# Seven unit loads begin during memory clearing, and the preparation of units in the first four pairs is dealt out anew

## The reference

```
for t in range(S):                                   # S = 768
    y[:, :, t] = einsum('bhd,bhde->bhe', r_t, state)
    Sa = einsum('bhde,bhe->bhd', state, a_t)
    state = state * w_t - outer(Sa, b_t) + outer(v_t, k_t)
x = y as (3072, 320)
g = h - tanh(h), h = x @ w_in (320 x 2048);   x = g @ w_out
out = sum over e of p[:, e] * (relu(x @ w1[e]) @ w2[e]),  p = probs / sum(probs)
```

## Time and profile before

| what | us |
|---|---|
| median of 3 runs | 1708.87 |
| the runs | 1700.08 to 1709.82 |
| the profiled execution | 1711.34 |
| its span on the core | 1709.6 |

### The profile page before, as it was taken

One profiled execution on the slowest core, in us unless ns is written; L12 is line 12 of the kernel. 1 busy time (PEld: TensorE's weight loads), 2 busy tenths in 40 slices (PEclk: granted clock), 3 DMA queues, 4 the chain that ended last, 5 costly groups with the idle time before them and its releaser, 6 DMA issues. The chain is left out here.

```text
span 1709.6 us, 37877 instructions
## 1 busy us (share of the span) xinstructions
PE 1494.2 (87%) x15888; PEld 1296.8 (76%) x15888; DVE 805.4 (47%) x1395; ACT 423.2 (25%) x859; POOL 403.9 (24%) x362
## 2 busy tenths in 40 slices
PE   0278476988989998899996969999999999999998
PEld 0266355876877786697795859999999999999998
DVE  5767844956855675493411133333333333333332
ACT  0023233333323323332432221111111111111111
POOL 5122354324323332231133341201010101010000
PEclk9988677999997998998998979999999999999999
DMA  7645475057046307403101051010101010100011
GB/s 196 195 107 148 131 221 163 4 144 210 27 105 172 104 5 200 109 5 99 27 1 35 10 167 34 0 34 0 34 0 34 0 34 0 34 0 0 0 46 46
DMA packets 83483, 123.06 MB, mean 72 GB/s; under 512 B 10016, under 2 KB 61472, under 8 KB 83360
## 3 DMA queue, kind: packets, MB, share of 16 engines
q1 hardware_dynamic: 83360, 121.27, 25.5%
HBM read 83.84 MB, written 37.40 MB: 71 GB/s over the span
## 5 line engine op out<-in xcount | busy, mean ns | idle before, releaser
L1330 PE MATMUL banks<-x2t,u 128*128 x1536 | 377.4, 393 | 8.6 <-POOL u L1297 8.6
L1340 PE MATMUL banks<-u,hid 128*128 128x320 f32 x2304 | 360.6, 309 | 0.0
L1340 PEld LDWEIGHTS banks<-u,hid 128*128 128x128 f32 x2304 | 349.0, 188 | 11.2
L1330 PEld LDWEIGHTS banks<-x2t,u 128*128 128x128 f32 x1536 | 284.1, 189 | 61.5 <-issue 8.8
L1395 DVE SCALAR_TENSOR_TENSOR hid<-banks,hid 128x512 fp32r<-128x512 f32 x192 | 132.8, 692 | 413.9 <-ACT hid L1365 413.9
L1365 ACT ACTIVATE hid<-banks 128x512 fp32r<-128x512 f32 x192 | 115.0, 599 | 581.5 <-PE banks L1330 581.5
L763 PE MATMUL banks<-xt,wi 128*128 128x512 f32 x768 | 197.0, 400 | 19.8 <-issue 12.4
L772 PE MATMUL banks<-wo,hid 128*128 128x320 f32 x1152 | 183.8, 309 | 5.7 <-POOL hid L1167 5.7
L772 PEld LDWEIGHTS banks<-wo,hid 128*128 128x128 f32 x1152 | 175.3, 188 | 14.1 <-POOL hid L1167 6.4
L763 PEld LDWEIGHTS banks<-xt,wi 128*128 128x128 f32 x768 | 142.3, 191 | 47.6 <-issue 21.0
L1167 POOL TENSOR_TENSOR hid<-gap,hid 128x512 fp32r<-128x512 f32 x96 | 123.7, 1288 | 223.5 <-ACT hid L903 223.2
(11 more groups left out here) (105 smaller groups left out, 1635.9 us busy)
## 6 DMA issues: line engine op xcount, KB each, us to landing
scaled_operands<-made SPq DMA_DIRECT2D x42, 520.8 KB
made<-kbaw SPq DMA_DIRECT2D x42, 520.0 KB
kb<-scaled_operands SPq DMA_DIRECT2D x24, 416.0 KB
raw<-w SPq DMA_DIRECT2D x8, 640.0 KB, 5.7
lam<-scaled_operands SPq DMA_DIRECT2D x24, 209.6 KB
raw<-w SPq DMA_DIRECT2D x8, 512.0 KB, 4.0
rt<-rvt SPq DMA_DIRECT2D x96, 40.0 KB
vt<-rvt SPq DMA_DIRECT2D x96, 40.0 KB
```

Of the source, the lines that this page charges most:

```text
L1330: mm = pe.matmul(p_up[f][:], u1[:, par, w, f * 128:(f + 1) * 128], xt[:, x, cols], start=(i == 0), stop=(i == 7))
L1340: mm = pe.matmul(p_dn[t][:, 0:D], hid[:, f, h, t * 128:(t + 1) * 128], u2[:, par, w, f, :], start=(f == 0 and i == 0), stop=(f == NFU - 1 ...
```

## The change

**Loads during clearing.** SP gets a program in the first block: the raw loads of units 0 to 6, in place of the loads of units 0 to 4 that stood at the head of `start`. Units 5 and 6 go into the memory of `nvmak` and of `kbn`, which their own stages write first in `mask_scores(0, 0)` and `save_natural(0, 0)`. These two therefore wait, the first time, until unit 5 or unit 6 has been stored. DVE clears a constant column in both.

**Slots.** Units 0 to 6 have slots of their own. Then a ring of five is used up to unit 16, and one of three from 17 on. In `start` SP now loads units 7 to 14 (before: 5 to 12).

**Preparation.** Pair 0 prepares units 10 to 13 and pair 1 prepares 14 and 15 (before: three each). Pairs from 3 on are as before.

**Inverse of chunk 1.** Its steps in pairs 2 and 3 are (0, 6, 7, 4, 6) and (3, 2, 6, 4, 6), 44 in all (before: (2, 3, 3, 2, 4) in each, 28 in all). The other 22 (before: 38) run after pair 3.

**Weight pieces.** `PIECES_FROM` is 4, so the pieces come in pairs 4 to 7 (before: 3 to 6), and `load_tokens(0)` moves behind the last pieces of pair 7 on SP.

```diff
+EARLY = RING + 2
-PIECES_FROM = 3
+PIECES_FROM = 4
+LAST_RAW = (15, 16)

 def slot(i):
-    return i % RING if i < 2 * NG else i % MADES
+    if i < EARLY:
+        return i
+    return (i - EARLY) % RING if i <= LAST_RAW[1] else (i - LAST_RAW[1] - 1) % MADES
...
 def prepared_in(p):
     if p < 2:
-        return list(range(FIRST + 3 * p, FIRST + 3 * p + 3))
+        return [[10, 11, 12, 13], [14, 15]][p]
 def loaded_in(p):
-    if p < 3:
-        return [[13, 14], [15], [16]][p]
+    if p < 4:
+        return [[], [15], [16, 17], [18]][p]
...
+            @block.sync
+            def _(sp):
+                for i in range(EARLY):
+                    sp.dma_start(raw_of(i)[0:PR, 0:WW + OP_LAM], kbaw[i, :, :]).then_inc(raw_op_in[i], 16)
...
             def start():          # SP
-                for i in range(RING):
-                    load_raw(i)
...
-                    if 0 < i <= 8:
-                        load_raw(i - 1 + RING)
+                    if 0 < i <= RING:
+                        load_raw(i - 1 + EARLY)
+                    if i >= 8:
+                        load_raw(i + 4)
+                load_raw(14)
...
             def pair(p):          # SP
-                if p == 2 * PPC - 1:
-                    load_tokens(0)
-                elif p % PPC == 0 and p >= 2 * PPC:
+                if p % PPC == 0 and p >= 2 * PPC:
                     load_tokens(c - 1)
...
                     raw_piece(2 * (p - PIECES_FROM) + 1)
+                if p == 2 * PPC - 1:
+                    load_tokens(0)
...
             def save_natural(p, j):
+                if p == 0 and j == 0:
+                    act.wait_ge(op_stored[RING + 1], 16)
             def mask_scores(p, j):
+                elif j == 0:
+                    dve.wait_ge(op_stored[RING], 16)
...
             def pair(p):          # DVE
-                spread = PPC - 2 <= p < PPC
+                steps = {2: (0, 6, 7, 4, 6), 3: (3, 2, 6, 4, 6)}.get(p, (0, 0, 0, 0, 0))
...
+                if p == 0:
+                    invert_decay(i[0])
                 sides(1)
+                if p == 0:
+                    prepare(i[1])
...
                 sides(2)
+                if p == 0:
+                    prepare(i[2])
...
+                if p == 0:
+                    prepare(i[3])
                 some(4)
                 update_state(p)
-                for k in i[2:]:
-                    prepare(k)
```

More of the change, by code:

```diff
@@ L186, in raw_of @@
             t = slot(i)
-            return made[:, t, :] if t < MADES else spare[:, t - MADES, :]
+            if t < MADES:
+                return made[:, t, :]
+            if t < RING:
+                return spare[:, t - MADES, :]
+            if t == RING:
+                return nvmak[:, :, :, :, :, :].rearrange("p j s a q t -> p (j s a q t)")[:, 0:MADE]
+            return kbn[:, :, :, :, :, :].rearrange("p k j a q e -> p (k j a q e)")[:, 0:MADE]
         def parts(i):
@@ L240, in _ @@
                     dve.memset(t[:, :, WW + OP_LAM::C + 1], 1.0).then_inc(set_v, 1)
+                for i in range(RING, EARLY):
+                    dve.memset(raw_of(i)[:, WW + OP_LAM::C + 1], 1.0).then_inc(set_v, 1)
                 dve.memset(rt[:], 0.0).then_inc(set_v, 1)
@@ L243, in _ @@
                 dve.memset(un[:], 0.0).then_inc(set_v, 1)
-                dve.wait_ge(set_v, 5)
+                dve.wait_ge(set_v, 7)
             @block.gpsimd
@@ L263, in _ @@
                 pool.wait_ge(set_p, 9)
-        raw_op_in = [sem(f"raw_operands_loaded{i}") for i in range(RING)]
-        op_stored = [sem(f"operands_stored{i}") for i in range(RING)]
+        op_stored = [sem(f"operands_stored{i}") for i in range(EARLY)]
         kb_in = [sem(f"scaled_kb_loaded{i}") for i in range(2)]
@@ L408, in raw_piece @@
                 if i < 2:
-                    last = 13 + i
+                    last = LAST_RAW[i]
                     sp.wait_ge(op_stored[slot(last)], 16 * uses(last))
@@ L1045, in pair, with some @@
                 finish = p > 0 and not drained(p - 1)
-                spread = PPC - 2 <= p < PPC
-                def some(n):
-                    if spread:
-                        inverse_steps(1, n)
+                steps = {2: (0, 6, 7, 4, 6), 3: (3, 2, 6, 4, 6)}.get(p, (0, 0, 0, 0, 0))
+                def some(k):
+                    inverse_steps(1, steps[k])
                 def sides(b):
@@ L1061, in pair @@
                     mask_ur(p - 1)
-                some(2)
+                some(0)
+                if p == 0:
+                    invert_decay(i[0])
                 sides(1)
-                for k in i[:1]:
-                    invert_decay(k)
-                some(3)
+                if p == 0:
+                    prepare(i[1])
+                elif i:
+                    invert_decay(i[0])
+                some(1)
                 sides(2)
@@ L1069, in pair @@
                     save_result(p - 1)
-                for k in i[1:2]:
-                    scan(k, 0)
-                    scan(k, 1)
-                some(3)
+                if p == 0:
+                    prepare(i[2])
+                elif i:
+                    scan(i[1], 0)
+                    scan(i[1], 1)
+                some(2)
                 sides(3)
@@ L1076, in pair @@
                     mask_scores(p + 1, 0)
-                some(2)
+                some(3)
                 if p + 1 < NP:
                     mask_scores(p + 1, 1)
-                for k in i[1:2]:
-                    invert_decay(k)
+                if p == 0:
+                    prepare(i[3])
+                elif i:
+                    invert_decay(i[1])
                 some(4)
                 update_state(p)
-                for k in i[2:]:
-                    prepare(k)
             def make_gap(c, f):
```

5 lines of the change are left out of this document (2 added, 3 removed).

## The result

The changed kernel takes **1712.89 us** (median of 20 runs, 1707.91 to 1724.46); the kernel before, on the same chip and in the same rounds, 1708.65 (20 runs, 1692.44 to 1718.61). The ratio is **1.0044, with a 95% interval from 1.0027 to 1.0062**: slower by some 7.5 us (the two medians by themselves lie 4.2 apart), and within the 1% that the prediction called no change. The profiled execution took 1712.49 us, its span is 1710.8.

What follows compares the result with a forecast made beforehand. It took the first MLP matmul's start as decisive, with the load queue pacing the start and DVE's inverse the stretch after pair 3; -15.2 + 16.4 = +1.2 us gave 1712.5 profiled, 1710 beside the median, range 1698 to 1720.

Steps and rivals of the forecast that it cites:

- 1, the start: Start: earlier raw loads, with two more in the queue, let the first mask begin at 49.8 instead of 51.03; -1.3 us.
- term 2: Pair 0: a fourth preparation comes in, two now lying between block rows where DVE waited for PE anyway; +0.1 us.
- term 3: Pair 1: the 3.7 us preparation behind its state update goes, one more diagonal passes through PE; -2.5 us.
- term 4: Pair 2: DVE's 2.78 us wait for a diagonal's copy goes, nine added inverse steps meet idle time; -3.0 us.
- 5, pair 3 and the tail: Pair 3 and the inverse behind it: added steps lengthen the pair, the tail loses 12.6 us; together -8.5 us.
- 6, pieces and tokens: Before the first MLP: pair 7's weight pieces and the tokens' load behind them delay its first matmul; +16.4 us.
- B: Rival, start: the queue is quicker than measured, engines set the pace, mask at 38.6; 1699 us, chance 0.12.
- C: Rival, pair 2: added inverse steps stand on the chain, losing its gain and costing up to 3 more; 1715, chance 0.17.
- D: Rival, start: no data moves before the first block ends, so the mask starts 3.9 us later; 1715, chance 0.09.

Runs made afterwards that it cites:

- e6: Changed kernel with units 2 and 3 instead of 5 and 6 loaded into the mask's and natural keys' memory; ratio to the kernel before 1.0035.
- e9: Kernel before with only its own five raw loads moved into the first block, during clearing; ratio to the kernel before 0.9923.
- e12: Kernel before with its five raw loads begun during clearing and the changed numbers of inverse steps; 1696.29 us, ratio to the kernel before 0.9921.
- e4: Changed kernel with its seven raw loads put back behind the clearing of memory, at the head of `start`; ratio to the kernel before 1.0080.
- e3: Changed kernel with the old numbers of inverse steps, 14 each in pairs 2 and 3; ratio to the kernel before 1.0104.
- e10: Changed kernel with pair 2's small loads of r issued ahead of its store and raw loads; ratio to the kernel before 1.0016.
- e1: Changed kernel with the weight pieces begun in pair 3 again instead of pair 4; ratio to the kernel before 1.0008.
- e2: Kernel before with only the weight pieces begun in pair 4 and the tokens' load behind them; ratio to the kernel before 1.0064.
- e11: e7 with the order of pair 2's transfers from e10; ratio to the kernel before 0.9914.
- e7: Changed kernel with the edits of e1 and e6 together; ratio to the kernel before 0.9955.

## Why the prediction was right, by its steps

The prediction had a gain of 15.2 us up to pair 4, paid back by 16.4 at the MLP. The trace has 11.4 and 15.5.

*1, the start (-1.3): right.* Measured -0.73 at the mask and at the inverse. The mechanism was the named one: the store of unit 5 had to leave the mask's memory, and the wait is longer than the 1.3 suggests, since without it the mask could have started at 39.57, 10.7 us sooner; e6 gives back 5.6 of them. The prediction put the early issue at 3.75 us. Held against all traces with the same start, it is 3.7 to 5.0 with five loads (e9, e12) and 2.5 to 3.7 with seven (e4).

*2 to 4, pairs 0 to 2 (together -5.4): mis-sized.* Measured, from each pair's start to the next, -2.5, +1.1 and 0.0, together -1.4. The failing steps are 3 and 4: they miss 6.6 us, and it is luck that term 2, forecast at +0.1, hides 2.6 of it.

In term 3 I took the 3.7 us of preparation behind a state update for time on the chain. They weren't. Without them pair 1 starts 3.7 sooner behind pair 0's update (0.63 against 4.32 us), which is the gain that term 2 shows, but from update to update it takes 23.90 us, 23.36 before. And pair 2 takes 22.01 in e12, where that preparation still stands behind pair 1's update, and 21.3 to 22.2 in the kernels without it. Pair 0 itself grew by 1.2 (from its start to its update 17.67 against 16.51), so the preparations between its block rows were not free. In pair 1 PE's waits for nothing that the profile shows also went from 2.50 us in one place to 3.65 in two; the prediction had no term for them.

In term 4 the nine added steps were to fall into DVE's idle time. They stand on the chain: from the mask of the second block row to the state update pair 2 takes 14.00 us, 11.86 before, and DVE waits for no other engine in it (e3). The wait of 2.78 for a diagonal's copy did go, and in its place PE waited 2.02 and DVE 2.71 for PE. Why PE waits there is open (e10).

*5, pair 3 and the tail (-8.5): right.* Measured -9.3: pair 3 grew by 2.7, forecast 4.1, and the tail lost 12.0, forecast 12.6. That it is the steps is shown by e3, that the pieces beside the inverse cost DVE about 5 us by e1 and e2 (5.4 and 4.8).

*6, pieces and tokens (+16.4): right.* Measured +15.5, with e2 giving 16.0 for this edit alone. From the `vt` loads of pair 7 (done at 273.24) to POOL's last piece it takes 14.2, where I had read 14.3 from pair 6. The tokens need 10.3 to the first matmul; 11.0 was forecast.

*Rivals.* B is out. The engines were as quick as it says, with PE's scores ready at 39.57 and B's mask at 38.6, but the store of unit 5 landed near 50, not before 45: the queue moved 210 and 229 GB/s from 0.82 to 25.16 and on to 50.30, near the 206 and 250 of the earlier trace rows and not the some 358 of the Trainium skill (DMA: Bandwidth & Descriptors, Specifications). C came half true: term 4 is lost, and the steps that outlast PE's and ACT's part of a block row are a reason for it (2.1 us), but pair 2 is no longer than before. D is out: data moved at once, since the first scan came at 5.43, and e4 shows the mask 2.6 later without the early issue.

*The whole.* The trace's +4.1 at the MLP lies just under the ratio's +7.5 (4.6 to 10.6). Pairs 5 to 7, with the same work, took 1.6 us more in the trace before (74.02 against 72.43); without that it would be +5.7, inside. The forecast of +1.2 was short by the missing part of terms 3 and 4. The two large terms, 5 and 6, were right, and the total stayed small because gains and loss cancelled; undoing the sixth and the reuse of memory while keeping the first and fifth gives e12.

## What to carry to other kernels

Before starting work later to clear a busy stretch, ask which chain then ends last: the pieces left DVE's inverse 5 us shorter and became the last thing before the MLP, for 16. Transfers into memory of a later stage only help if that memory is empty when the stage comes, so the units that leave first belong there, or none (e6 got back half, e9 and e12 avoid it). Steps put into an engine's idle time cost nothing only where that engine would still be waiting when they end: a pair's total idle time, 6.0 us here, doesn't say that for a single gap. When a change bundles parts of both signs, its near-zero result hides a faster kernel: time the parts alone.

## What the hardware showed that I had not expected

- PE stood for 0.9 to 3.0 us at fixed places of its instruction stream without a semaphore to wait for, more of them in one arrangement of the same work than in another.
- **A single pair takes up to 4 us more from one execution to the next, and the granted clock is not all of it.** In pairs 5 to 7 PE stands once for ACT's copy of a diagonal, which in ACT's order comes behind the high parts of two weight pieces, and ACT waits for their transfers. By stage, in the kernel before, pairs 6 and 7, which do the same:

```profile
235.32:262.78 27.46, 19.83 (x422) 15.75 (x420) 12.06 (x22) 9.73 (x24) 12.87 (x13) 0.75 0.68 192
262.78:286.04 23.26, 17.60 (x422) 14.00 (x420) 12.35 (x21) 9.83 (x24) 12.59 (x13) 0.85 0.83 241
```

  and from the timelines of ACT and PE, in pair 6 and, in the last line, in pair 7:

```profile
244.46 0.63 ACT L846 ACTIVATE wi<-spare 128x512 fp32r<-128x512 f32 x1 [2.34 <-DMA spare<-w_out]
...
246.04 0.28 ACT L809 ACTIVATE ld<-banks 128x128 f32<-128x128 f32 x1
...
246.46 0.66 PE L509 MATMUL banks<-made 104*32 104x32 f32 x32 [6.72 <-ACT ld L809]
...
271.78 0.85 PE L509 MATMUL banks<-made 104*32 104x32 f32 x30 [4.58 <-ACT ld L809]
```

  Of the 4.2 us between the two pairs, 2.1 are this wait; and with more of the pair at the lower of the clock's two levels (1.2 GHz) PE is busy 2.2 longer. In all fourteen traces the three pairs 6 of 27.4 to 27.8 us have a wait of 6.7 to 7.4, the other pairs 6 and 7 one of 4.5 to 6.2 at 23.1 to 24.4 us. Pair 5 took 27.0 to 27.9 in three traces, at a granted clock of 0.68 or 0.69, and 23.3 to 25.5 at 0.73 to 0.79 in the others. What makes the pieces late is not shown.

  The clock by itself is seen in pair 1 of e11 and of e7, which have the same work there:

```profile
102.66:128.55 25.89, 22.00 (x446) 17.29 (x435) 12.15 (x21) 6.88 (x19) 6.18 (x7) 0.67 0.54 159
```

```profile
101.48:125.14 23.66, 18.69 (x445) 14.53 (x435) 12.14 (x21) 6.87 (x19) 6.19 (x7) 0.78 0.59 173
```

  DVE, ACT and POOL are busy as long, PE 3.3 us longer at 0.67 than at 0.78, and the pair is 2.2 longer. Pair 1 of the kernel before took 23.36 at 0.78 and in e2, with the same work, 20.02 at 1.00. Reading one trace of each kernel for a difference of 4 us can mislead, as e9 did.
- PE's first eight MLP matmuls take 3.75 us after 23.43 us of idle time as after 7.32, at a granted clock of 0.50 both times; the longer wait cost nothing beyond itself.
- Moving the tokens' load to the end of SP's pair, harmless while the pieces come last, costs 2.1 to 2.9 us where they don't (from pair 7 to the MLP 9.74 in e1, 10.34 in e11 and 10.58 in e7; 7.67 in e12 and e9).
